# Threshold search of the overlapped routings in five rounds of 90 thresholds, with routing steps, input turns and the last stage's end placed elsewhere

## The reference, cut to what matters

```python
logits = x @ w_gate                      # 2304 x 8
order = np.argsort(-logits.flatten())    # best (token, expert) pairs first
for idx in order:
    tok, e = idx // E, idx % E
    if assigned[tok] >= 0 or counts[e] >= cap: continue
    assigned[tok] = e; counts[e] += 1
for e in range(E):
    mask = assigned == e
    out[mask] = np.maximum(x[mask] @ w1[e], 0) @ w2[e]
h = x @ w_in                             # the dense layer
y = h * sigmoid(h) @ w_out
```

## Time and profile before

| | |
|---|---|
| time, median of 3 runs | 928.77 us (927.79 to 928.84) |
| profiled execution, its own time | 928.7 us |
| its span | 927.0 us |
| TensorE (PE) busy | 857.6 us, 93% |
| VectorE (DVE) busy | 496.3 us, 54% |
| ScalarE (ACT) busy | 345.6 us, 37% |
| GpSimd (POOL) busy | 298.6 us, 32% |
| mean granted TensorE clock | 0.971 |

### The profile page before, as it was taken

How to read it: one execution, slowest core, us unless ns; L and a number is a source line. 1 busy time by engine, 2 the same in 40 slices (tenths; PEclk the granted TensorE clock), 3 DMA queues, 4 the chain that set the end, 5 groups by cost and what they waited for, 6 DMA issues and landing times.

```text
span 927.0 us, 17883 instructions
## 1 busy us (share of the span) xinstructions
PE 857.6 (93%) x6792; PEld 796.7 (86%) x6792; DVE 496.3 (54%) x1685; ACT 345.6 (37%) x814; POOL 298.6 (32%) x298
## 2 busy tenths in 40 slices
PE   7999999932999999999999999999999999999996
PEld 6999999931988898889889888988898889899995
DVE  6666666556657457455745561656457455732110
ACT  5666656502324333423432242324333432433221
POOL 1422222414125223522522262326123522523222
PEclk9999999955999999999999999999999999999998
DMA  6666666303303213030312120303212030321000
GB/s 159 154 149 149 154 155 151 105 14 117 92 1 118 67 49 92 26 112 4 117 55 60 53 65 1 125 3 116 68 48 92 27 115 1 117 69 46 1 1 34
DMA packets 117253, 71.43 MB, mean 77 GB/s; under 512 B 61616, under 2 KB 103600, under 8 KB 117168
## 3 DMA queue, kind: packets, MB, share of 16 engines
q1 hardware_dynamic: 114192, 60.85, 24.0%
q0 software_dynamic: 2976, 9.44, 3.3%
HBM read 60.83 MB, written 9.44 MB: 76 GB/s over the span
## 4 chain that ended last, share of the span: by engine, by line
PE 65%; DVE 10%; ACT 1%; issue 1%; DMA 1%; POOL 1%; SPq 0%; DVEq 0%; POOLq 0%
PE hp L1033 11%; PE hp L1035 10%; PE hp L1034 10%; PE acc L1092 6%; PE acc L1094 6%; PE acc L1093 6%; PE acc L1033 4%; PE acc L1034 4%; PE acc L1035 4%; PE rt L977 3%; DVE test L1214 1%; DVE h_raw L1438 1%; ACT gate L1172 1%; DVE closing L1281 1%; DMA rows<-x_rows,tokens 1%
## 5 line engine op out<-in xcount | busy, mean ns | idle before, releaser
L960 POOL TENSOR_TENSOR h_l<-h_raw,h_h 128x256 fp32r<-128x256 f32 (+1 forms) x128 | 107.8, 842 | 266.5 <-ACT h_h L1180 266.3
L1033 PE MATMUL hp<-xy_h,res_h 128*128 128x256 f32 (+1 forms) x512 | 155.1, 303 | 0.8
L1034 PE MATMUL hp<-xy_l,res_h 128*128 128x256 f32 (+1 forms) x512 | 151.7, 296 | 0.0
L1035 PE MATMUL hp<-xy_h,res_l 128*128 128x256 f32 (+1 forms) x512 | 151.7, 296 | 0.0
L1438 DVE TENSOR_TENSOR h_raw<-hp,gate 128x256 f32<-128x256 f32 (+1 forms) x128 | 58.2, 455 | 173.8 <-ACT gate L1172 173.8
L946 POOL TENSOR_TENSOR wb_l<-wb_raw,wb_h 128x512 fp32r<-128x512 f32 x64 | 87.5, 1369 | 177.3 <-ACT wb_h L1126 175.8
L1172 ACT ACTIVATE gate<-hp 128x256 f32<-128x256 f32 (+1 forms) x128 | 52.3, 409 | 178.2 <-PE hp L1035 175.1
L1092 PE MATMUL acc<-res_h,h_h 128*128 128x512 f32 x288 | 116.9, 406 | 0.0
L1093 PE MATMUL acc<-res_l,h_h 128*128 128x512 f32 x288 | 113.5, 394 | 0.0
L1094 PE MATMUL acc<-res_h,h_l 128*128 128x512 f32 x288 | 113.5, 394 | 0.0
L1033 PEld LDWEIGHTS hp<-xy_h,res_h 128*128 128x128 f32 x512 | 97.3, 190 | 6.0 <-issue 2.3
(11 more groups left out here) (212 smaller groups left out, 1800.3 us busy)
## 6 DMA issues: line engine op xcount, KB each, us to landing
wa_raw<-in_moe_w_dram SPq DMA_DIRECT2D x64, 256.0 KB, 4.1
wb_raw<-in_moe_w_dram SPq DMA_DIRECT2D x64, 256.0 KB, 3.1
q_rows<-in_q_dram SPq DMA_DIRECT2D x32, 128.0 KB, 3.5
k_rows<-in_k_dram SPq DMA_DIRECT2D x32, 128.0 KB, 2.7
v_rows<-in_v_dram SPq DMA_DIRECT2D x32, 128.0 KB, 2.4
stage<-in_moe_w_in_dram SPq DMA_DIRECT2D x8, 512.0 KB, 4.6
x_rows<-x_rows_sb SPq DMA_DIRECT2D x16, 256.0 KB, 4.2
stage<-in_moe_w_out_dram SPq DMA_DIRECT2D x8, 512.0 KB, 4.6
```

Source lines behind the costliest of these rows:

```text
L960: pool.tensor_tensor(h_l[:, cols], h_raw[:, cols], h_h[:, cols].bitcast(FP32), ALU.subtract).then_inc(g_low, 1)
L1033: nc.tensor.matmul(out_, weights_h, cols_h, start=start, stop=False)
L1034: nc.tensor.matmul(out_, weights_h, cols_l, start=False, stop=False)
L1035: return nc.tensor.matmul(out_, weights_l, cols_h, start=False, stop=stop)
```

## The change

It has five parts.

1. For j = 1 to 7 the search has 5 rounds of 90 thresholds in place of 6 of 40: three on the upper bits (18 of a 31-bit key and the carry), two on the lower 13. The compare on VectorE becomes 128x1800 elements (was 128x800). The first routing keeps its 6 rounds of 40. GpSimd makes the second set of thresholds ahead of the experts.
2. `setup` moves from slot 0 to slot 3, and the hooks move: the search from slots 5 to 21 to slots 8 to 24, the steps after it from 23, 25, 29, 30, 32 to 26, 30, 34, 36, 38. The gather (`fetch`) moves from slot 29 to slot 34, the weight halves of the next expert from slots 29, 31, 33, 35 to 32, 34, 36, 38.
3. The four turns of the next input all come in slot 45, in four different banks (three there and the last in slot 47 when the batch has 384 tokens); before they were two in slot 45 and two in slot 46, in two banks.
4. In the very last stage the steps b14 and b15 are done together, output tile by output tile.
5. The wait for the last scatter moves from the end of GpSimd's program to the end of SyncE's.

```diff
-SETUP_AT = {FIRST[2 * _j - 2]: _j for _j in range(1, E)}
-HOOK_LIST = {_j: [FIRST[2 * _j - 2] + _n for _n in (5, 6, 8, 9, 11, 12, 14, 15, 17, 18, 20, 21, 23, 25, 29, 30, 32)]
+KW = [40] + [90] * (E - 1)
+LOW_BITS = [16] + [13] * (E - 1)
+SETUP_AT = {FIRST[2 * _j - 2] + 3: _j for _j in range(1, E)}
+HOOK_LIST = {_j: [FIRST[2 * _j - 2] + _n for _n in (8, 9, 12, 13, 16, 17, 20, 21, 23, 24, 26, 30, 34, 36, 38)]
              for _j in range(1, E)}
...
 for _j in range(1, E):
-    X_AT[AT[2 * _j - 1, "b", FT2 - 3]] = [(_j, 0), (_j, 1)]
-    X_AT[AT[2 * _j - 1, "b", FT2 - 2]] = [(_j, 2), (_j, 3)]
+    _late = BATCH[_j - 1][1] > 2 * P
+    X_AT[AT[2 * _j - 1, "b", FT2 - 3]] = [(_j, _c) for _c in range(DC - _late)]
+    if _late:
+        X_AT[AT[2 * _j - 1, "b", FT2 - 1]] = [(_j, DC - 1)]
...
-        _n = max(FIRST[_s - 1] + 13, HOOK_LIST[_w // FT1][2 * ROUNDS] + 4) + 2 * _f
+        _n = max(FIRST[_s - 1] + 13, HOOK_LIST[_w // FT1][CLOSE[_w // FT1]] + 6) + 2 * _f
...
-            return tp if c % 2 == 0 else acc[DC - 1]
+            if c == 0:
+                return hp[(A_NO[2 * j, 0] - 1) % 2]
+            if c == 2:
+                return acc[DC - 1]
+            return tp if c == 1 or BATCH[j - 1][1] > 2 * P else acc[2]
...
+            sp.wait_ge(scattered, 16 * TILES_OUT[-1])
...
-            pool.wait_ge(scattered, 16 * TILES_OUT[-1])
...
+                if s == len(STAGES) - 1 and f >= FT2 - 2:
+                    if f == FT2 - 2:
+                        return
+                    fs = [FT2 - 2, FT2 - 1]
+                    pe.wait_ge(g_low, FT2 * k + FT2 - 1)
...
                 for t in range(tiles):
+                    for b in fs:
+                        o = FT2 * DM + DM * b
+                        m = slice(COLS * (b % 3) + P * t, COLS * (b % 3) + P * (t + 1))
+                        if t == 0 and b > fs[0]:
+                            pe.wait_ge(g_low, FT2 * k + FT2)
```

More of the change, by code:

```diff
@@ L785, in experts @@
         test = sb("test", [P, NT * GT + P - GT], BF16)
-        at_least = test[:, 0:NT * KW].rearrange("p (t k) -> p t k", k=KW)
+        at_least = [test[:, 0:NT * KW[j]].rearrange("p (t k) -> p t k", k=KW[j]) for j in range(E)]
         onehot = test[:, 0:NT * GT].rearrange("p (t k) -> p t k", k=GT)
         earlier = test[:, 0:2 * NT * E].bitcast(FP32).rearrange("p (t e) -> p t e", e=E)
-        reached = sb("reached", [KW, E])
+        reached = sb("reached", [KW[-1], E])
         hit = sb("hit", [P, 1], BF16)
@@ L898, in _, with thresholds @@
             pool.memset(test[:], 0.0).then_inc(rungs_ready, 1)
-            for n, step in enumerate(STEPS):
-                pool.iota(rungs[:, n, :], pattern=[[step, KW]], base=step, channel_multiplier=0,
-                          allow_small_or_imprecise_dtypes=True).then_inc(rungs_ready, 1)
+            def thresholds(j):
+                for n, step in enumerate(STEPS[j][0:HIGH_ROUNDS]):
+                    pool.iota(rungs[j][:, n, :], pattern=[[step, KW[j]]], base=step, channel_multiplier=0,
+                              allow_small_or_imprecise_dtypes=True).then_inc(rungs_ready, 1)
+            thresholds(0)
             pool.memset(ones[:], 1.0).then_inc(init_seq, 1)
@@ L1008, in part @@
                 last.then_inc(pe_part, 1)
-            def turn_x(j, c, bank):
-                if c == 0:
-                    pe.wait_ge(gathered, (j + 1) * (16 * GR))
-                if j >= 1 and c == 1:
-                    pe.wait_ge(y_low, j * DC)
-                elif j >= 1 and c >= 2:
-                    pe.wait_ge(x_low, j * DC + c - 1)
-                for a in range(GR):
-                    last = nc.tensor.transpose(bank[:, GT * a:GT * (a + 1)], rows[:, a, P * c:P * (c + 1)],
-                                               ident[0:GT, 0:GT])
-                last.then_inc(xt_done, 1)
             def bank_free(no):
@@ L1029, in bank_free, with turn_x @@
                     pe.wait_ge(g_done, FT2 * STAGES[s][1] + f + 1)
+            def turn_x(j, c, bank):
+                if c == 0:
+                    pe.wait_ge(gathered, (j + 1) * (16 * GR))
+                    if j >= 1:
+                        bank_free(A_NO[2 * j, 0] - 2)
+                        pe.wait_ge(y_low, j * DC)
+                if j >= 1 and c == 3 and bank is tp:
+                    pe.wait_ge(x_low, j * DC + 2)
+                for a in range(GR):
+                    last = nc.tensor.transpose(bank[:, GT * a:GT * (a + 1)], rows[:, a, P * c:P * (c + 1)],
+                                               ident[0:GT, 0:GT])
+                last.then_inc(xt_done, 1)
             def product(out_, weights_h, weights_l, cols_h, cols_l, start, stop):
@@ L1232, in setup @@
                 need(key_now)
-                key_now = step(nc.vector.tensor_scalar(half[:], bits[:], 16, None, ALU.arith_shift_right))
+                key_now = step(nc.vector.tensor_scalar(half[:], bits[:], LOW_BITS[j], None, ALU.arith_shift_right))
                 need(liked_now)
@@ L1404, in _ @@
             dve.wait_ge(weight_ready, 1)
-            setup()
+            setup(0)
             nc.vector.memset(zeros[:], 0.0)
@@ L1412, in _ @@
             dve.wait_ge(init_done, 1)
-            for h in range(HOOKS - 1):
+            for h in range(HOOKS[0] - 1):
                 after(0, h)
@@ L1427, in _ @@
                 if n in SETUP_AT:
-                    setup()
+                    setup(SETUP_AT[n])
                 if kind == "a" and stage == "A":
```

98 lines of the change are left out of this document (52 added, 46 removed).

## The result

The changed kernel takes 895.49 us (median of 4 runs, 895.17 to 895.74) against 928.68 us for the kernel before (4 runs): 33.2 us less, a ratio of 0.9644 with a 95% interval of 0.9628 to 0.9661. The profiled execution took 895.57 us itself.

What follows compares the result with a forecast made beforehand. From 229 us on the kernel was taken to be TensorE's work plus its stalls. Gains of 34.0 us less added waits of 12.8 gave 21.2 us, so 928.7 became 907.5 us, range 899 to 919 us (8 in 10).

Steps and rivals of the forecast that it cites:

- `setup` out of slot 0: Start of a stage: a2 no longer waits for a0's `h_l` behind `setup`; 11.2 us gained over 7 routings.
- `row_pair`, `row_counts`: Routing steps after the search: more slots end TensorE's waits for both; 8.2 and 2.5 us gained.
- turns: Input transposes in slot 45: twelve in one go cost about 0.9 us, 0.7 us less in six routings; 4.3 us gained.
- seam: From stage A to M: a counting part of 0.60 us covers a0's wait for the low halves; 2.0 us gained.
- end: Last scatters: tiles complete earlier, last issue waits for its own tile, 0.8 us gained; moved wait taken at 0 (0 to 0.5).
- slots 3 to 9: Work behind `setup`, with `wb_l` against `wa_l` in slot 7, makes `hit` late in slot 9; 5.6 us lost (0 to 9.8).
- slots 17 to 20: Third compare, behind the key-joining operations and a0's `h_l`, ends late for slot 20; 2.1 us lost (0 to 3).
- slots 21 to 23: Two slots hold 2.9 us; `h_raw` of a3, `base` and the compare need 3.3; 2.7 us lost (0 to 4).
- slots 34 to 38: `full` waits up to 1.9 us for GpSimd, so slot 38's part comes 0.4 late; 2.4 us lost (0 to 5).
- rival 1: VectorE and GpSimd block each other more than reckoned, sharpest at slot 17 delaying b0: 913.5 to 919.5 us; chance 0.2 beyond 913.
- Rival 2: Nothing new waits on TensorE, only the gains count: 894.7 us, 901 with half the added waits; chance 0.12 below 901.
- Rival 3: Gather issued in slot 34 leaves rows late for slot 45: slower, 932 us from 6.5 us on; chance 0.05 with unseen like it.

Runs made afterwards that it cites:

- The run with forty: Changed kernel with 6 rounds of 40 thresholds in its new places, in place of 5 of 90: 906.18 us, 0.9751 of the kernel before.

## Why the prediction was wrong

By its own steps, in us. "Measured" is from distances in the trace of the changed kernel unless a run is named.

| step | predicted | measured |
|---|---|---|
| one search round | 5.0 | 5.0 (1.2 more, by steps left out, stands in the row "not in the prediction") |
| `setup` out of slot 0 | 11.2 | 11.2, the stall is gone |
| `row_pair`, `row_counts` | 10.7 | 10.7, both gone; by another cause in part |
| turns | 4.3 | 3.6 (run: 3.6) |
| seam | 2.0 | 2.0, gone |
| end | 0.8 | 3.1 (run: 2.7) |
| slots 3 to 9 | -5.6 | -1.7 |
| slots 17 to 20 | -2.1 | 0 |
| slots 21 to 23 | -2.7 | -2.1 |
| slots 34 to 38 | -2.4 | -1.7 |
| not in the prediction | 0 | about 3 |
| together | 21.2 | 33.2 |

**The step that failed is the sum of added waits, 12.8 us for 5.5**, and in it first "slots 3 to 9". That is 7.3 of the 12 us; the end (2.3) and what the prediction left out (about 3) make up the rest, less 0.7 at the turns. The block was as described: `wb_l` delayed the `wa_l` of slot 7 by 1.04 us. What was wrong is the reckoning of everything else: "757.4, then `hit` 757.8", 14.84 us after the stage's start. Less the block's 1.04 the measured `hit` would have ended at 654.27, 13.94 after the start. `setup` begins 6.4 us into the stage (646.72) and not 6.8, and an `h_l` costs the queue 0.36 us (652.95 to 653.31) and not 0.5. So there were 0.9 us of slack more than reckoned, and they swallowed nearly the whole block: `hit` ended at 655.31 where TensorE wanted it at 655.26. The wait is 0.16 to 0.29 us in six routings and 0.54 in the fifth. The run with `wb_l` in slot 8 shows the block's whole price, 1.5 us in all. So the size of the block was right (0.6 to 1.3 reckoned), and the slack in front of it was put at nothing.

**Slots 17 to 20.** GpSimd and VectorE at slot 17, and TensorE at slot 20:

```profile
670.98 0.77 POOL L978 TENSOR_TENSOR h_l<-h_raw,h_h 128x256 fp32r<-128x256 f32 x1 [5.97 <-ACT h_h L1210]
```

```profile
671.21 2.43 DVE L1246 SCALAR_TENSOR_TENSOR test<-rungs,base,key 128x1800 bf16<-128x1800 f32 x1
```

```profile
673.53 0.39 PE L1123 MATMUL acc<-res_h,h_l 128*128 128x512 f32 x1
673.76 0.66 PE L994 MATMUL rt<-choice,test 128*128 128x8 bf16 x20
```

The compare lasts 2.43 us and not 2.09, since the `h_l` got in ahead of it, as the prediction held against rival 1. It ends at 673.64, 4.2 us after slot 17 starts on TensorE (669.41), and the 20 matmuls start at 673.76 with nothing lost: the fit is 0.1 us wide. The prediction had the end at 4.4 to 4.75 us and charged 0.35; the matmuls' own time, 4.4, was right.

**Slots 21 to 23 and 34 to 38** were right in kind and place, and about a quarter too large. In the second the small operation that waits for GpSimd is the one behind `full`, which took 0.51 us:

```profile
700.50 1.28 POOL L964 TENSOR_TENSOR wb_l<-wb_raw,wb_h 128x512 fp32r<-128x512 f32 x1
700.60 1.21 DVE L1385 TENSOR_SCALAR penalty<-full 128x8 f32<-128x8 f32 x1
```

**The end** was mis-sized by 2.3 us, nearly all of it in "the moved wait I take at 0". Its range, 0 to 0.5, was narrower than the profile allowed: after the last issue the span went on for 6.6 us, and no row told what they were. It was worth 1.9 us in the profile. The other half, the tiles, brought 1.1 or so and not 0.8.

**The turns** were right in mechanism: twelve cost 1.03 us with the restart behind them and not 0.9, which leaves 0.6 a period and not 0.7.

**Not in the prediction:** about 3 us. One us of it is TensorE's granted clock at the first period's start, read from the windows of the changed kernel:

```profile
233.00:234.00 1.00, 1.00 (x8) 1.00 (x8) 0.11 (x1) 0.00 (x0) 0.00 (x0) 0.91 0.00 0
```

The third figure from the end is the granted clock, 0.91 of the full 2.4 GHz here; the kernel before had 0.50 (the 1.2 GHz level) in this stretch and the next, so about 1 us more was lost there. TensorE had been mostly idle in the first routing ahead of it, in both kernels. In two other executions of the changed kernel the same stretch had 0.59 and 0.82, and over all runs here, with `setup` in slot 0 or 3, the full clock came back between 232.9 and 235.9 us. So this microsecond belongs to the two executions and not, as far as anything shows, to the change. The other 2 us are 0.2 to 0.3 a period. After a small matmul the next step is 0.08 to 0.09 us longer; the round that went had two of them, 0.17 a period, which the prediction's distances left out, and the seam's wait had one behind it (691.69 to 691.88, 0.07). The run with forty, which has both again, is longer by just these steps; a few hundredths stay open.

**The rivals.** Rival 2 came true but for 0.8 us, by luck, with two errors that cancel: waits of 5.5 us that it denied, and gains that neither it nor the forecast had. Rival 1 is real as a mechanism, 0.90 us for b0 when a plain compare is put there. The changed kernel is full of such holds, one of them on an `h_l` of GpSimd, but b0 isn't hit and none costs TensorE more than the few tenths above:

```profile
676.92 2.09 DVE L1246 SCALAR_TENSOR_TENSOR test<-rungs,base,key 128x1800 bf16<-128x1800 f32 x1
677.35 2.25 POOL L978 TENSOR_TENSOR h_l<-h_raw,h_h 128x256 fp32r<-128x256 f32 x1 [0.94 <-ACT h_h L1210]
```

Rival 3 is 4.8 us away from its threshold, 3.1 with the slowest gather seen. A chance of 0.12 for rival 2 was too low: four added waits, each a few tenths over a limit that was itself reckoned from sums of up to ten rows, were all taken as real, and their errors had the same sign.

## What to carry to other kernels

Reckon a queue of an engine by the distances from start to start (0.36 us for an `h_l`) and not by the durations (0.45), or ten rows make a microsecond that isn't there, and an added wait of a few tenths that comes out of such a sum may be none at all. Where a step stands in the queues weighs more than what it costs: the same wider compares made this kernel 12 us slower at the old places (about 7 of it by the clock) and 33 us faster at the new ones, and moving four steps and one weight half by one or two slots gave 4 to 5 us more. A stall can cost more than its length: look at the granted clock of the stretch behind it, which no list of waits shows. What no row explains isn't worth nothing: where the span goes on for microseconds behind the last issue, leave it a range as wide as that.

## What the runs showed of the hardware that was not expected

- Where the last wait for a scatter stands matters: 6.6 us from the last issue to the end of the span with it on GpSimd, 4.7 us with it on SyncE.
- The matmul that waited for gathered rows (96 tokens of 512 values) started 3.1 to 3.2 us after the start of the last of the gather's issues eleven times, and once 4.7 us after it.
- After stalls of TensorE of 2.0 to 2.7 us at a stage's start the granted clock fell to the 1.2 GHz level in four of seven periods, at about 1.7 us each; after stalls of 0.9 to 1.6 us in the kernel before it did not.
- The hold between VectorE and GpSimd goes both ways, and the later one waits for most of the other's length: a compare of 2.09 us became 3.17 beside a `wb_l` of 1.28, an `h_l` of 0.77 became 2.25 beside a compare that had begun 0.43 us before.
- After a one-column or eight-column matmul the next product's first step is 0.08 to 0.09 us longer, behind each of the ten search steps of a period.
